# Six of eight weight transfers of expert 1 wait for the rows of the second tile

## What is computed

```python
def _attn_ref(q, k, v, f):                 # 4 batches, 8 heads, 576 tokens, head 64
    cum = np.cumsum(np.log(np.clip(f, 0.0001, 1.0)), axis=-1)
    scores = q @ k.T / 8 + cum[..., :, None] - cum[..., None, :]   # causal mask, softmax
    return softmax(scores) @ v

def _moe_ref(x, expert_emb, tau, w1, w2):  # 2304 tokens, 512 wide, 8 experts, 1024 hidden
    logits = xn @ en.T / tau               # rows of x and of expert_emb normalized
    expert_idx = np.argmax(logits, axis=1)
    gate_w = probs[np.arange(N), expert_idx]
    for e in range(E):
        mask = expert_idx == e
        h = np.maximum(x[mask] @ w1[e], 0.0)
        out[mask] = gate_w[mask, None] * (h @ w2[e])
```

## Time and profile before

| | us |
|---|---|
| median of 3 runs | 910.94 |
| lowest and highest of them | 904.73 and 911.35 |
| the profiled execution, its own time | 905.14 |
| its span, first to last instruction | 903.6 |

### The profile page before, as it was taken

How to read it: one execution, slowest core, us unless ns; L and a number is a source line. 1 busy time by engine, 2 the same in 40 slices (tenths; PEclk the granted TensorE clock), 3 DMA queues, 4 the chain that set the end, 5 groups by cost and what they waited for, 6 DMA issues and landing times.

```text
span 903.6 us, 16352 instructions
## 1 busy us (share of the span) xinstructions
PE 862.4 (95%) x5025; PEld 709.3 (79%) x5026; DVE 575.3 (64%) x1723; ACT 403.8 (45%) x708; POOL 293.9 (33%) x459
## 2 busy tenths in 40 slices
PE   6999999999997899999999999969999999999995
PEld 5788777777776788888888888858888888888884
DVE  7777888888876576757487767536652264425643
ACT  2455645646652553535265535205551254324541
POOL 7344455345435422233133222222122121122120
PEclk7999999999999999999999999989999999999998
DMA  4334444544522854334265544306652162516100
GB/s 133 95 103 128 128 123 131 152 141 126 169 63 72 296 172 170 124 129 160 98 206 172 169 156 136 113 26 227 217 187 95 35 226 69 189 41 223 46 26 23
DMA packets 59244, 119.63 MB, mean 132 GB/s; under 512 B 11934, under 2 KB 20638, under 8 KB 59204
## 3 DMA queue, kind: packets, MB, share of 16 engines
q1 hardware_dynamic: 49620, 96.93, 33.2%
q0 software_dynamic: 9440, 22.18, 7.5%
q10 hardware_dynamic: 144, 0.04, 0.0%
HBM read 104.13 MB, written 17.99 MB: 135 GB/s over the span
## 4 chain that ended last, share of the span: by engine, by line
PE 80%; DVE 11%; DMA 3%; issue 3%; SPq 1%; POOL 1%; ACT 0%; POOLq 0%; DVEq 0%; ACTq 0%
PE ps L636 27%; PE ps L607 26%; PE ps L445 8%; PE ps L432 5%; PE ps L440 4%; DVE ps L868 3%; PE ps L450 2%; PE ps L403 2%; PE ps L415 2%; PE ps L416 1%; PE ps L404 1%; DVE kA L840 1%; DMA k_raw<-in_k 1%; DVE kA L828 1%; DVE hot L1029 1%
## 5 line engine op out<-in xcount | busy, mean ns | idle before, releaser
L1089 DVE TENSOR_TENSOR wlo<-stage,whi 128x1024 fp32r<-128x1024 f32 x136 | 160.0, 1221 | 31.8 <-ACT whi L703 30.3
L703 ACT CAST whi<-stage 128x1024 fp32r<-128x1024 f32 x136 | 133.6, 1057 | 0.0
L768 ACT ACTIVATE h_s<-ps 128x512 f32<-128x512 f32 x44 | 26.3, 598 | 219.9 <-PE ps L607 219.9
L432 PE MATMUL ps<-probT,v_s 128*65 128x448 f32 (+4 forms) x384 | 103.3, 391 | 3.5 <-POOL probT L1299 3.4
L636 PE MATMUL ps<-whi,hT_hi 128*128 128x512 f32 x352 | 99.5, 404 | 0.0
L636 PE MATMUL ps<-whi,hT_lo 128*128 128x512 f32 x352 | 99.1, 403 | 0.0
L607 PE MATMUL ps<-whi,xT_hi 128*128 128x512 f32 x352 | 94.9, 392 | 3.0 <-DVE xT_lo L1195 3.0
L607 PE MATMUL ps<-whi,xT_lo 128*128 128x512 f32 x352 | 95.2, 392 | 0.0
L636 PE MATMUL ps<-wlo,hT_hi 128*128 128x512 f32 x352 | 95.0, 392 | 0.0
L607 PE MATMUL ps<-wlo,xT_hi 128*128 128x512 f32 x352 | 94.9, 392 | 0.0
L868 DVE CUSTOM_DVE_ANT_0 ps<-ps,maskf 128x576 f32<-128x576 f32 (+4 forms) x160 | 75.3, 510 | 20.6 <-PE ps L404 19.2
(11 more groups left out here) (223 smaller groups left out, 1626.6 us busy)
## 6 DMA issues: line engine op xcount, KB each, us to landing
stage<-in_moe_w SPq DMA_DIRECT2D x128, 512.0 KB, 4.3
q_raw<-in_q SPq DMA_DIRECT2D x64, 144.0 KB, 3.0
k_raw<-in_k SPq DMA_DIRECT2D x64, 144.0 KB, 3.1
v_s<-in_v SPq DMA_DIRECT2D x32, 162.5 KB, 2.3
x<-o_rows SPq DMA_DIRECT2D x8, 512.0 KB, 3.9
kB<-cum_hl SPq DMA_DIRECT2D x64, 2.2 KB, 1.7
table<-entry POOLq DMA_INDIRECT x44, 2.5
table<-tinit SPq DMA_DIRECT2D x2, 288.0 KB
```

The source lines that it names most:

```text
L432: mm = pe.matmul(ps[0:D + 1, OT_AT + lo:OT_AT + hi], v_s[h % 3][:, t, :], probT[:, col:col + hi - lo], start=(t == 0), stop=(t == QT - 1 o ...
L703: act.copy(whi[b][:, c, :], stage[:, c, :]).then_inc(w_hi[c], 1)
L768: act.activation(h_s[:, 0:512], h_ps[0], ACT.Relu).then_inc(h_relu[0], 1)
L1089: dve.tensor_tensor(wlo[b][:, c, :], stage[:, c, :], whi[b][:, c, :].bitcast(F32), ALU.subtract).then_inc(w_lo[c], 1)
```

## The change

SP issues chunks 0 and 1 of expert 1 after the first gather, as before, then waits for the second gather, and then issues chunks 2 to 7. What follows in SP's program stays in its order behind them.

```diff
             sp.wait_ge(xg_in, 16)
-            load_weights(0, 1, 1)
+            load_weights(0, 1, 1, range(2))
+            sp.wait_ge(xg_in, 32)
+            load_weights(0, 1, 1, range(2, CH))
             sp.wait_ge(g_ent_out, 16 * GT)
             sp.wait_ge(first_rows, 2)
             sp.dma_start(ent_tab[0][:, 8:].rearrange("p (s c) -> p s c", c=4),
```

## The result

| | us |
|---|---|
| changed kernel, median of 10 runs | 916.55 (913.94 to 919.33) |
| kernel before, median of 10 runs | 909.39 (904.73 to 911.90) |
| ratio, 95% interval | 1.0084 (1.0062 to 1.0107) |
| profiled execution of the changed kernel, its time and span | 915.34 and 913.8 |

The change makes the kernel 0.84% slower, some 7.6 us of 909. In this trace attention ended later: the first gather is issued at 287.33 instead of 286.00, and the edit acts only behind it.

What follows compares the result with a forecast made beforehand. TensorE, 80% of what ended last, was taken as the bound. Third gather +4.25 (gain already counted) and clock +1.75 made +6.0 us: 911.1 against the profiled 905.14, 916.9 in terms of the median; range 906 to 921.

Steps and rivals of the forecast that it cites:

- Second gather: POOL's gather for tile 1: issue stays at 297.90, landing at 301.4 (301.2 to 301.8) instead of 303.92.
- Gain of 1.72 in every bound: TensorE's wait for the second gather's rows in tile 1 disappears, saving all of its 1.72 us.
- SP's six issues, 4.2 us: Issuing chunks 2 to 7 from 301.5 takes SP 4.2 us, moving the token table's load from 298.73 to 305.7.
- Drain, 7.7 us at 408 GB/s: On the DMA engines, six chunks, 3.15 MB, flow until 310.3; the table behind them lands at 311.4 instead of 304.6.
- POOL, 5.2 us from table to gather: POOL still needs 5.2 us from table landing to third gather's issue, which moves from 309.77 to 316.6.
- Third gather's landing, 5.5 us: Running among expert 2's chunks, the gather takes 5.5 us and lands at 322.1 (320.1 to 322.6).
- rival 1: Third gather lands in 3.5 us as in light traffic and the clock holds: +2.3 us, 913.2; chance 0.17.
- The wait in tile 2: TensorE arrives at 316.1 and stands until 322.1 for the third gather; rows turned 4.25 us later than before.
- The clock, 1.75 us: After TensorE's stand in the second tile, 3.5 us of work at half clock loses 1.75 us (bounds 0 and 3).
- Rival 2: Token table doesn't queue behind the weights and lands at 307.8: net -1.3 to -0.3 us, at best -1.72; chance 0.12.
- What is hidden: The six later chunks cost nothing in ACT's and DVE's splits: chunk 2 lands near 304.8, chunk 7 near 311.3.
- cover of 3 us: Chunk 7's slack: the relu behind the splits comes due on ACT at 313.1, PE needs it by 315.7; over 3 us.

Runs made afterwards that it cites:

- changed_again: The changed kernel measured once more, nothing altered, for a second trace; ratio 1.0072 to the kernel before.
- hold_expert2: Changed kernel, but SP holds expert 2's chunks until the third gather has landed; ratio 1.0032 to the kernel before.
- none_early: Changed kernel, but all eight chunks wait for the second gather; ratio 1.0102 to the kernel before.
- five_table_first: Changed kernel, but five chunks go at once, then the token table, then the wait for the second gather and three chunks; ratio 0.9987 to the kernel before.
- keep_clock: Changed kernel with 120 small matmuls in TensorE's second tile before its wait for the third gather; ratios 1.0109 and, repeated, 1.0070 to the kernel before.
- table_pool: Changed kernel, but POOL loads expert 0's token table on its own queue instead of SP behind the chunks; ratio 1.0042 to the kernel before.
- table_first: Changed kernel, but SP loads expert 0's token table before its wait for the second gather and chunks 2 to 7; ratio 0.9956 to the kernel before.
- table_first_again: The kernel of table_first measured once more, for a second trace; ratio 0.9982 to the kernel before.
- five_early: Changed kernel, but five chunks go at once and three wait for the second gather; ratio 1.0014 to the kernel before.

## Why the prediction was right, step by step

The forecast was 916.9 us against a measured 916.55, and the mechanism is the one forecast: the gain in tile 1, the table behind six chunks, POOL behind the table, a larger wait in tile 2, then the clock. The match of the absolute time is in part luck: the added time was forecast at 6.0 us and is 7.2 by the medians, 7.6 by the ratio and 8.6 by the front stretch, while the median of before, taken as 910.94, is 909.39 over ten runs. The two misses cancel. Of the added time itself the forecast was +4 to +7.5 us, so the measured one lies at or just beyond the upper end.

- *Second gather.* Forecast to land at 301.4, 15.4 us from the first gather; measured 15.3 (302.65 - 287.33). Its issue stayed 11.9 us behind the first gather's, as said.
- *Gain of 1.72 in every bound.* Right. From the first gather, the rows were turned at 17.96 us before; changed_again has 16.23, a gain of 1.73:

```profile
305.55 0.60 PE L447 MATMUL ps<-ident,xg 128*128 128x128 f32 x4
...
327.91 1.11 PE L447 MATMUL ps<-ident,xg 128*128 128x128 f32 x4 [8.35 <-DMA xg<-x,ent_next]
...
343.40 0.60 PE L447 MATMUL ps<-ident,xg 128*128 128x128 f32 x4
```

  There TensorE comes to its first rows 8.05 us after the first gather, as before. In the changed kernel's first trace it came there after 6.42, its small matmuls before having run at full clock (3.30 us for 56 instead of 4.93); it turned the second rows at 15.36, 2.60 us sooner than before, and could have done so sooner still: it waited 0.59 us, since the gather's issue stands behind POOL's seven issues.
- *SP's six issues, 4.2 us.* Mis-sized: 2.95 (302.66 to 305.61), on the average 0.42 for those of L311 and 0.52 for those of L315 instead of 0.73 and 0.68. It didn't matter, since the transfers and not the issues set the table's landing.
- *Drain, 7.7 us at 408 GB/s; table 10.0 us after the second gather.* Mis-sized by 1.3: it took 11.3. The 3.15 MB flowed in about 8.8 us, 358 GB/s on the average, and the table landed 1.3 us after them instead of 1.1 (the forecast's own rows give 1.2); the flow had single microseconds at 401 to 410 and a weak stretch:

```profile
305.00:306.00 1.00, 1.00 (x7) 0.83 (x5) 0.57 (x1) 0.33 (x1) 0.00 (x0) 1.00 1.06 410
306.00:307.00 1.00, 1.00 (x10) 0.99 (x9) 0.00 (x0) 0.99 (x1) 0.00 (x0) 1.00 1.13 298
307.00:308.00 1.00, 1.00 (x6) 0.78 (x5) 0.91 (x1) 0.66 (x2) 0.00 (x0) 1.00 0.69 240
```

  This stage view is of the changed kernel; hold_expert2 and changed_again have the same dip (264 and 301 GB/s), none_early hardly (340 once, else 385 to 408). What makes it is open.

  The 358 GB/s of the page (the Trainium skill, DMA: Bandwidth & Descriptors, "Where 436 GB/s comes from"), which the forecast set aside, met this stretch's mean. As a limit the traces don't bear it out: single microseconds here reach 410, and none_early's 4.2 MB flowed at some 390.
- *POOL, 5.2 us from table to gather.* 5.21 (313.99 to 319.20).
- *Third gather's landing, 5.5 us.* Mis-sized by 1.05: 6.55, and 6.6 to 7.2 in the eight other traces with full traffic (five_table_first, with fewer chunks in flight, had 5.1). The forecast took a value between two rows when the row of full traffic, 6.0, was at hand; hold_expert2 shows that the traffic makes the difference (3.35). This also rules out rival 1.
- *The wait in tile 2.* Forecast 6.0, measured 8.91, the two sizes above and the early arrival being the difference.
- *The clock, 1.75 us.* 1.99 in the trace (15.81 against 13.82): the work at the low clock lasted about 4.0 us instead of 3.5. In the total, see keep_clock.
- *Rival 2, the table doesn't queue.* Not so in SP's queue. Nor on POOL's: in table_pool the load took 5.75 us, not 2.1, about as long as behind three chunks in SP's queue. table_first is this rival made true, and its times come out on the faster side, but not as priced (-1.72 at best): -4.0 us in the first series, -1.6 in the second, and the traces of both are slower in the front stretch.
- *What is hidden.* From the first gather, chunk 2 was split from 18.7 us instead of 19.0, chunk 7 from 26.5 instead of 25.3. The relu behind it ran from 314.77 to 315.36; TensorE needed it by 316.28. Of the cover of 3 us that was named 0.9 was left, and it held; in table_first it did not, by 0.23 us.

## What to carry to other kernels

A wait added in a queue delays everything behind it, and the small item may be the dear one: here a 32 KB table behind 3.15 MB of weights held GpSimd for 10.4 us, and TensorE waited 8.9 us for the gather behind it, where the change had saved 1.7 to 2.6. In a case like this, try the small loads that others wait for ahead of the bulk, and let the bulk wait for them. When a change shifts a bulk transfer, look up which gather or table now falls into its traffic.

## What was not expected of the hardware

- A small load's time to landing depended on the traffic, and no run shows that it depended on the queue: 1.8 to 2.2 us (SP, light), 5.3 us (SP, behind three chunks), 3.7 (five_table_first) to 6.5 us (POOL, among the chunks of expert 1), 7.8 to 8.9 us (SP, behind six or eight).
- A gather of 128 rows took 3.35 to 3.8 us in light traffic and 6.55 to 7.2 us in full. Its issue on GpSimd took 1.07 us in light traffic, and 1.08 (the changed kernel) to 1.96 us (none_early) in full.
- The clock fell at quite different places of an idle time. In table_first it fell in one of 2.72 us (in table_first_again in one of 2.24), while the 1.56 us of before had no low clock behind it:

```profile
320.00:321.00 1.00, 0.00 (x0) 0.00 (x0) 1.00 (x2) 0.00 (x0) 0.00 (x0) 1.00 1.01 383
321.00:322.00 1.00, 0.59 (x3) 0.59 (x4) 0.73 (x2) 0.00 (x0) 0.00 (x0) 0.53 1.05 418
322.00:323.00 1.00, 1.00 (x7) 1.00 (x6) 0.00 (x0) 0.44 (x1) 0.00 (x0) 0.50 1.04 396
```

  In the changed kernel it fell about 3 us into the idle time, in changed_again about 5 us into it (1.00 in 323 to 324, 0.74 in 324 to 325, the idle time having begun at 319.6), and in five_early, after 3.83 us of idle time, only about a microsecond into the work behind it.
- Much of the scatter lies elsewhere: in the traces of all kernels the first gather is issued between 286.0 and 289.3 us, before the edits act, and from the first turn of rows in the second layer to the last product of the profile it is 287.0 to 290.1 us.
